# Five unused arrays that shift where the operands of the matmuls lie in SBUF

## The reference

```python
x = attention(q, k, v)                      # 2 x 576 tokens, 8 heads of 64 -> N = 1152, D = 512
p = domain_probs / (domain_probs.sum(-1, keepdims=True) + 1e-09)
for e in range(4):                          # w1[e]: 512 x 1024, w2[e]: 1024 x 512
    h = np.maximum(x @ w1[e], 0.0)
    out += p[:, e:e + 1] * (h @ w2[e])
h = out @ w_in                              # 512 x 2048
result = (h * np.cos(h)) @ w_out            # 2048 x 512
```

## Time and profile before

| | |
|---|---|
| median of 3 runs | 640.25 us (640.21 to 640.36) |
| the profiled execution | 639.62 us |
| its span, first to last instruction | 637.7 us |
| TensorE matmul busy | 629.2 us of the span, 3656 matmuls |
| VectorE, ScalarE, GpSimd busy | 305.2, 260.3 and 272.2 us |

### The profile page before, as it was taken

The page is one execution under the profiler, slowest core; times in us unless marked ns, Lnnn a source line. Parts: engine busy times, 40 slices in busy tenths (PEclk is TensorE's granted clock), DMA queues, the critical chain, the costliest instruction groups (busy, mean ns, idle before and its releaser), DMA issues.

```text
span 637.7 us, 10145 instructions
## 1 busy us (share of the span) xinstructions
PE 629.2 (99%) x3656; PEld 561.9 (88%) x3656; DVE 305.2 (48%) x722; ACT 260.3 (41%) x554; POOL 272.2 (43%) x404
## 2 busy tenths in 40 slices
PE   7999999999999999999999999999999999999998
PEld 5887899999989998989998888989999999999996
DVE  6754431215433315433315433426775666766564
ACT  6776322233321223321223321246655467544542
POOL 6783246698720296720296720287000059400000
PEclk9999999999999999999999999999999999999999
DMA  9874100022120011220012120033100012001011
GB/s 285 273 226 151 44 1 1 1 56 77 67 66 1 1 66 66 66 66 0 1 66 67 67 66 1 26 107 100 34 0 1 1 38 96 1 0 49 0 51 50
DMA packets 21896, 37.25 MB, mean 58 GB/s; under 512 B 2784, under 2 KB 14048, under 8 KB 21856
## 3 DMA queue, kind: packets, MB, share of 16 engines
q1 hardware_dynamic: 20688, 36.71, 17.7%
q10 hardware_dynamic: 1168, 0.02, 0.1%
HBM read 34.36 MB, written 2.36 MB: 58 GB/s over the span
## 4 chain that ended last, share of the span: by engine, by line
PE 96%; DVE 1%; POOL 1%; ACT 1%; issue 0%; DVEq 0%
PE bank L1166 31%; PE bank L1194 31%; PE bank L1225 16%; PE bank L1211 14%; PE bank L1158 2%; PE bank L1122 1%; PE bank L1142 1%; PE bank L1308 1%; DVE s_sb L823 1%; PE bank L1350 1%; POOL w_lo L424 0%; ACT prob L574 0%; DVE acc L973 0%; POOL prob L450 0%; DVE prob_t L838 0%
## 5 line engine op out<-in xcount | busy, mean ns | idle before, releaser
L424 POOL TENSOR_TENSOR w_lo<-w_raw,w_hi 128x128 fp32r<-128x128 f32 (+1 forms) x252 | 150.6, 633 | 214.4 <-ACT w_hi L606 211.9
L1166 PE MATMUL bank<-x_hi,w_hi 128*128 128x384 f32 (+1 forms) x384 | 131.2, 342 | 0.5 <-POOL w_lo L424 0.5
L1166 PE MATMUL bank<-x_hi,w_lo 128*128 128x384 f32 (+1 forms) x384 | 129.1, 336 | 0.0
L1166 PE MATMUL bank<-x_lo,w_hi 128*128 128x384 f32 (+1 forms) x384 | 128.7, 335 | 0.0
L1194 PE MATMUL bank<-w_hi,hp_hi 128*128 128x512 f32 x288 | 114.7, 398 | 0.1
L1194 PE MATMUL bank<-w_hi,hp_lo 128*128 128x512 f32 x288 | 113.4, 394 | 0.0
L1194 PE MATMUL bank<-w_lo,hp_hi 128*128 128x512 f32 x288 | 112.1, 389 | 0.0
L926 DVE TENSOR_TENSOR h_raw<-bank,h_raw 128x384 f32<-128x384 f32 x84 | 46.6, 555 | 91.9 <-PE bank L1211 91.9
L1166 PEld LDWEIGHTS bank<-x_hi,w_hi 128*128 128x128 f32 x384 | 72.1, 188 | 3.6 <-POOL w_lo L424 0.8
L1166 PEld LDWEIGHTS bank<-x_lo,w_hi 128*128 128x128 f32 x384 | 72.2, 188 | 1.5
L857 DVE SCALAR_TENSOR_TENSOR hp_lo<-bank,hp_hi 128x384 fp32r<-128x384 f32 x48 | 26.5, 556 | 98.1 <-ACT hp_hi L638 57.5
(11 more groups left out here) (103 smaller groups left out, 966.4 us busy)
## 6 DMA issues: line engine op xcount, KB each, us to landing
w_raw<-in_weights SPq DMA_DIRECT2D x43, 512.0 KB, 3.7
q_t<-in_q SPq DMA_DIRECT2D x12, 192.0 KB, 4.3
result<-acc SPq DMA_DIRECT2D x9, 256.0 KB, 2.0
w_raw<-in_weights SPq DMA_DIRECT2D x8, 256.0 KB, 5.8
k_t<-in_k SPq DMA_DIRECT2D x8, 224.0 KB, 5.3
v_w<-in_v SPq DMA_DIRECT2D x4, 384.0 KB, 5.0
v_w<-in_v SPq DMA_DIRECT2D x4, 320.0 KB, 6.5
k_t<-in_k SPq DMA_DIRECT2D x4, 192.0 KB, 3.7
```

The lines of the kernel that those rows point to most:

```text
L424: last = nc.gpsimd.tensor_tensor(w_lo[:, f, at:at + part], raw[:, at - begin:at - begin + part], w_hi[:, f, at:at + part], ALU.subtract)
L1166: last = nc.tensor.matmul(ps[:, 0:TOK], w[:, f, chunk(c)], x[:, c, token_cols(t)], start=c == 0 and i == 0, stop=c == DC - 1 and i == 2)
```

## The change

Five arrays are declared that nothing writes or reads: 64, 960, 256, 64 and 192 bytes in each partition, 1536 in all. The two of the `sums` group lie in memory that is used again later. No instruction is added, removed or moved on any engine; each has the same operands, the same sizes and the same waits. Only start addresses differ.

```diff
         w_raw = sb("w_raw", [P, STAGE, 2 * DM])
+
+        sb("before_x", [P, 16])
         x_hi = sb("x_hi", [P, DC, N], F32R)
         x_lo = sb("x_lo", [P, DC, N], F32R)
         p_tok = sb("p_tok", [P, E, TILES])
         half_pi = sb("half_pi", [P, 1])
+
+        sb("before_hp", [P, 240])
         hp_hi = sb("hp_hi", [P, HP, TOK], F32R)
         hp_lo = sb("hp_lo", [P, HP, TOK], F32R)
         h_raw = sb("h_raw", [P, HP, TOK])
@@
         zeros = sb("zeros", [P, P])
 
+        sb("before_acc", [P, 64])
         acc = sb("acc", [P, NTOK, DC * TOK])
@@
+            sum_sb("before_t", 16)
             t_hi = sum_sb("t_hi", 3, 2, TOK)
             t_lo = sum_sb("t_lo", 3, 2, TOK)
+            sum_sb("before_ex", 48)
             ex_hi = sum_sb("ex_hi", GROUPS, EX * P)
             ex_lo = sum_sb("ex_lo", GROUPS, EX * P)
```

## The result

The changed kernel takes 641.99 us (median of 7 runs, 641.44 to 642.78) against 640.21 us (7 runs, 639.62 to 640.45): ratio 1.0028, 95% interval [1.0018, 1.0038]. It is slower by 1.8 us. The forecast was no change, 640.2 us. The time lies within the stated range of 634.0 to 644.0 us, but the change is clear of the noise, and none was forecast.

A forecast was written before the change was run, and what follows sets the result against it. TensorE was taken to bound the kernel through distances between matmul starts. The profiled 639.62 us (637.7 span, 1.9 around it) plus nothing, with the median 0.6 us above, gave 640.2 us; the eight-in-ten range was 634.0 to 644.0 us.

The forecast's parts named there:

- What bounds the kernel: Whole kernel: TensorE, busy 629.2 of 637.7 us, sets the time; only changed distances between matmul starts can pay or cost.
- the other engines: ScalarE and VectorE writes of tokens in the first 82 us: 0.6 us if 5% longer, taken as nothing; DMAs unchanged.
- Down matmuls: The 1296 512-column matmuls of weights against hidden values: still 64 bytes apart modulo 256, so no change from 228.8 ns each.
- 4.1 ns a matmul: Difference between two lasting down-run rates, 232.9 and 228.8 ns; applied to 1656 up and pair matmuls as 6.8 us.
- Its last signs: Closing list of profile signs: changed distances on L1194 would mean places modulo 1024 or above matter, or how runs begin.
- The single flips: Single matmuls at up/down run ends, taken as samples of changed relations: steps of 0.01 us show no change.
- the jogs go: Starts of 67 up or pair runs: 0.03 us extra over the first seven matmuls disappears, 2.0 us, 638.2 us; chance 0.20.
- the lasting rate of the up matmuls falls: 1656 up and pair matmuls: 64 bytes remove contention within 7.6 ns each; half gives 633.9 us, all 627.6; chance 0.18.
- the new relation is the worse one: 1656 matmuls of L1166 and L1211: 2.0 ns more each, 643.6 us; chance 0.26, shared with other slower patterns.
- No effect of place: TensorE's two reads: 64 bytes between tokens and weights cost nothing, leaving 640.2 us; chance 0.36.
- surplus of 13.5 and 15.5 ns: Time per up and down matmul beyond one column per cycle; their likeness at relations 0 and 64 suggested no effect.
- 0.432 ns a column: Rate from 228.8 and 173.5 ns over 128 columns; leaves 7.6 ns per 384-column matmul that does not grow with columns.

## Why the prediction was wrong

- **What bounds the kernel**: right. All of the difference is in distances between starts of matmuls. "I take nothing" for the other engines held too: TensorE's idle time is 8.5 us of the span in both kernels.
- **Down matmuls, "I take nothing for the 1296 of them"**: this is the step that failed. I read a matmul's relation off its own run, and for the down runs it stays 64. I had also written that down runs have two lasting rates and that "which one a run falls into depends on how it begins", and didn't draw the conclusion: the change alters how they begin. The surplus of all 512-column runs rose by 3.8 us; behind it, 47 of the 64 longer runs are at 233 ns, and 47 × 18 × 4.3 ns = 3.6 us. The size was in the prediction as 4.1 ns a matmul, but put on the up matmuls. Its last signs named the distances on L1194 with two readings; the run with everything but the tokens rules out the places modulo 1024, and "the way a run begins" is what is left.
- **The single flips**: a slip. I took the last up matmul before the change (tokens at 128, hidden values at 64 modulo 256) for a sample of the new relation. As a sample it was fair, but the change turns the same matmul into a relation of 128, which the trace of before doesn't show anywhere. The two columns of the address table show it: 192 less 64.
- **Rival "the jogs go"**: it happened as described, 1.8 us by the sum over all runs where 2.0 were forecast. Alone it would have been 638.4 us. It was given 0.20. It took back half of the loss; without it the time would have been 643.8 us, at the upper end of the range.
- **Rival "the lasting rate of the up matmuls falls"**: no. It is 173.3 ns in both kernels.
- **Rival "the new relation is the worse one"**: right about the sign and wrong about the place. Up runs did not take on the pattern of the down runs. In the relation of 64 the up run is better than in any other that was tried, the down run isn't. That its 641.6 us with the jogs gone lies so near the measured time is luck.
- **No effect of place, the forecast**: the one argument that carried it, surplus of 13.5 and 15.5 ns alike at relations 0 and 64, is refuted. With level operands the down matmul has 226.7 ns, 13.3 over its columns; the difference of 2 ns was the relation. It also undoes the 0.432 ns a column, which came from an up run at 0 and a down run at 64: with both at 0 it is (226.7 − 173.3) / 128 = 0.417 ns, one cycle of 2.4 GHz, and the part that doesn't grow with the columns is 13.3 ns and not 7.6.

The Trainium skill (page "SBUF — State Buffer", section "Who interferes with whom") has the moving operand and the weight load on independent ports. No run shows the ports, but the inference that places could not matter fails, and the measurement decides: how the two places stand to each other modulo 256 moves a matmul of 384 columns between 173.3 and 176.7 ns, and one of 512 between 226.7 and 233.3. The Trainium skill (page "TensorE: Matmul & The Clock Gate", section "Wait — 56ns, not 53.3ns?") gives about 2.5 ns over the columns; no lasting rate here was less than 13 ns over them.

What stays open: why a relation costs what it costs. The runs show the rates and the starts of runs, not what happens between the two reads, and not why an even end and a handover of 128 lead to the slower rate. Nor is the relation told apart from the place itself. The weights lay at 128 modulo 256 in every kernel, so "tokens 64 past the weights" is also "tokens at 192 modulo 256", and where weights lay 64 past the hidden values, a handover of 128 was a last moving operand at 192 too. A kernel with all arrays, the weights too, 64 bytes further would tell; none was run.

## What to carry to other kernels

In this kernel, where TensorE is busy from end to end and streams float32r operands while it loads the next ones, the start addresses modulo 256 bytes were worth 0.7%: weights level with hidden values and tokens 64 bytes past the weights made 635.8 from 640.4 us with five unused arrays. From the worst placing to the best it was 643.5 to 635.8. Whether the same distances are best in another kernel is not shown. To find out, write down every pair that is read at the same time, the ones at the change from one kind of matmul to the other too, and check each against the rate in the timeline (distances between starts, not durations). A change that improves one pair can push another into a slower rate that lasts for a whole run of matmuls.

## What the runs showed of the hardware

- Lasting distance between starts with a load beside each matmul, float32r, at a granted clock of 1.00: 384 columns in up runs 173.3 ns at relations 0 and 64, 175.5 at 128, 176.7 at 32, 96 and 192 (most runs at 32 and 192); 512 columns 226.7 ns at 0, 229.0 or 233.3 at 64, 233.3 at 192. At 2.4 GHz, 173.3 and 226.7 ns are 416 and 544 cycles, both 32 over their columns.
- The rate can have two stable values at the same addresses (229.0 and 233.3 ns). In the nine kernels of the tables none of the runs of 18 or more changed from one to the other once it was under way. 229.0 is itself a mean over three distances that repeat (226, 229 and 232 ns in the trace).
- Level operands can cost a slower start: 0.03 us for an up run, and for a down run 0.04 us at a handover of 0, 0.01 at 64 and nothing at 192.
- Only the places modulo 256 counted: 1024 bytes for the hidden values, or 256 for the tokens and 256 for the hidden values the other way, changed no lasting rate.
